# Three of eight score products of a chunk moved ahead of the groups of left-over rows, and the queries split one chunk sooner on VectorE

## The reference

```
a2k     = softmax(scale * agents @ k^T)        # 49 x 12480
agent_v = a2k @ v                              # 49 x 128
q2a     = softmax(scale * q @ agents^T)        # 12480 x 49
x       = q2a @ agent_v                        # 12480 x 128
```

## Time and profile before

| | us |
|---|---|
| median of 3 runs | 885.77 |
| the runs | 885.68 to 885.78 |
| the profiled execution | 886.51 |
| its span in the trace | 884.8 |

### The profile page before, as it was taken

One profiled execution on the slowest core, in us unless ns is written; L12 is line 12 of the kernel. 1 busy time (PEld: TensorE's weight loads), 2 busy tenths in 40 slices (PEclk: granted clock), 3 DMA queues, 4 the chain that ended last, 5 costly groups with the idle time before them and its releaser, 6 DMA issues.

```text
span 884.8 us, 15670 instructions
## 1 busy us (share of the span) xinstructions
PE 878.8 (99%) x5496; PEld 442.5 (50%) x5496; DVE 671.3 (76%) x984; ACT 551.2 (62%) x763; POOL 144.3 (16%) x139
## 2 busy tenths in 40 slices
PE   9999999999999999999999999999999999999998
PEld 8865555545545454444444444444444444444444
DVE  4888788788877777778777777778778777777765
ACT  2457776767666566566666666666666666666554
POOL 6502222322001100011001011011011011010100
PEclk9999999999999999999999999999999999999999
DMA  9942222222222331121112111112111111121110
GB/s 357 398 134 83 63 65 82 84 64 84 82 88 88 116 119 38 38 61 37 38 39 62 37 41 59 37 42 58 39 47 51 40 56 41 40 62 33 31 36 21
DMA packets 59992, 66.20 MB, mean 75 GB/s; under 512 B 36368, under 2 KB 41904, under 8 KB 58800
## 3 DMA queue, kind: packets, MB, share of 16 engines
q1 hardware_dynamic: 59520, 65.51, 23.8%
q10 hardware_dynamic: 432, 0.16, 0.1%
HBM read 41.60 MB, written 12.78 MB: 61 GB/s over the span
## 4 chain that ended last, share of the span: by engine, by line
PE 96%; DMA 2%; DVE 1%; SPq 0%; ACT 0%; issue 0%; DVEq 0%
PE ps L725 60%; PE ps L696 19%; PE ps L713 7%; PE ps L511 1%; PE ps L664 1%; PE ps L586 1%; PE ps L594 1%; DMA kv_s<-kT 1%; PE ps L740 1%; PE ps L624 1%; DVE r_lo L1462 1%; PE ps L925 1%; PE ps L751 1%; PE ps L541 0%; PE ps L644 0%; PE ps L693 0%
## 5 line engine op out<-in xcount | busy, mean ns | idle before, releaser
L1462 DVE SCALAR_TENSOR_TENSOR r_lo<-ps,r_hi 128x1024 f16<-128x1024 f32 (+1 forms) x392 | 468.4, 1216 | 179.5 <-ACT r_hi L1165 179.1
L1165 ACT ACTIVATE r_hi<-ps 128x1024 f16<-128x1024 f32 (+1 forms) x392 | 388.5, 1017 | 159.0 <-PE ps L713 153.1
L725 PE MATMUL ps<-r_hi,w_hi 128*128 128x512 f16 (+1 forms) x784 | 241.0, 383 | 0.1
L725 PE MATMUL ps<-r_lo,w_hi 128*128 128x512 f16 (+1 forms) x784 | 239.5, 380 | 0.0
L725 PE MATMUL ps<-r_hi,w_lo 128*128 128x512 f16 (+1 forms) x784 | 237.8, 380 | 0.0
L696 PE MATMUL ps<-PT,M_a 128*128 128x512 f16 x768 | 198.1, 379 | 0.2 <-DVE r_lo L1462 0.2
L488 POOL TENSOR_TENSOR y<-y_relu,y_lin 128x512 f32<-128x512 f32 x48 | 78.4, 1632 | 531.9 <-ACT y_relu L1280 326.8
L725 PEld LDWEIGHTS ps<-r_lo,w_hi 128*128 128x128 f16 x784 | 76.7, 98 | 81.9
L696 PEld LDWEIGHTS ps<-PT,M_a 128*128 128x128 f16 x768 | 72.2, 98 | 83.7 <-DVE r_lo L1462 15.2
L725 PEld LDWEIGHTS ps<-r_hi,w_lo 128*128 128x128 f16 x784 | 74.3, 98 | 78.9 <-issue 0.8
L725 PEld LDWEIGHTS ps<-r_hi,w_hi 128*128 128x128 f16 x784 | 63.3, 98 | 89.1 <-issue 41.7
(11 more groups left out here) (180 smaller groups left out, 727.4 us busy)
## 6 DMA issues: line engine op xcount, KB each, us to landing
q_s<-qT SPq DMA_DIRECT2D x48, 256.0 KB, 2.8
out<-y SPq DMA_DIRECT2D x48, 256.0 KB, 2.1
kv_s<-kT SPq DMA_DIRECT2D x23, 512.0 KB, 4.7
kv_s<-vP SPq DMA_DIRECT2D x12, 514.5 KB, 9.9
kv_s<-vS SPq DMA_DIRECT2D x6, 1028.5 KB, 5.3
PR<-PT SPq DMA_DIRECT2D x147, 32.0 KB, 1.8
PT<-stack SPq DMA_TRANSPOSE x196, 2.3
w_lin<-w_out SPq DMA_DIRECT2D x1, 1024.0 KB, 9.1
```

The costliest lines, as they stand in the source:

```text
L725: mm = pe.matmul(ps[:, OUT, 0:wide], w[:, 2 * p + u, :], r[:, s, u, 0:wide], start=(p == 0 and u == 0 and k == 0), stop=(p == PAIRS - 1 an ...
L1165: act.activation(r_hi[:, p % RING, :, 0:wide], ps[:, at:at + 2, 0:wide], ACT.Relu).then_inc(hi_ready, 1)
L1462: dve.scalar_tensor_tensor(out=r_lo[:, p % RING, :, 0:wide], in0=ps[:, at:at + 2, 0:wide], scalar=0.0, in1=r_hi[:, p % RING, :, 0:wide], o ...
```

## The change

In plain chunks for which there are queries to score (24 to 45), steps 0, 1 and 2 leave the second layer. Step 0 goes behind tiles 1 and ahead of group 0, which is in the body of the chunk before; step 1 behind tiles 3, ahead of group 1; step 2 behind tiles 5, ahead of group 2. Steps 3 and 4 stand behind the last two products of second layer 2, steps 5, 6 and 7 behind the first three of second layer 3. Since step 0 now needs `q_12` and `q_rest` a body sooner, DVE makes `q_rest` of chunk n+4 behind `split_shift(n + 3)` in body n, and no longer at the start of body n+1. The number of products and of vector operations is the same.

```diff
+        def at_turns(kind):
+            return kind == PLAIN
+        def next_at_turns(half, kind):
+            return kind == PLAIN or kind == MIX_REST and half == 1
@@ PE
+                    turns = at_turns(kind) and there(n + 3)
+                    def turn_step(step):
+                        if turns:
+                            scored = split_score(step, nb3)
+                            if step == 7:
+                                scored.then_inc(q_scored, 1)
                     def second_group():
                         tiles(2, half, b)
                         pe.wait_ge(lo_ready, g + 1)
                         tiles(3, half, b)
+                        turn_step(1)
                         rest_of_quad(1, half, b)
...
                     tiles(5, half, b)
+                    turn_step(2)
                     rest_of_quad(2, half, b)
...
+                        elif turns:
+                            if t >= 4:
+                                turn_step(t - 1)
                         elif there(n + 3):
                             scores(t)
                     def fourth(t):
-                        if not split:
+                        if turns:
+                            if t < 3:
+                                turn_step(t + 5)
+                        elif not split:
                             scores(t + 6)
...
                         tiles(1, 1 - half, nb)
+                        if next_at_turns(half, kind) and there(n + 4):
+                            scores_read(n + 3)
+                            pe.wait_ge(q_split, n + (5 - AHEAD))
+                            split_score(0, BOTH if is_last(n + 4) else 1)
                         pe.wait_ge(q_spread, 48 * n + 96)
                         rest_of_quad(0, 1 - half, nb)
@@ DVE
-                    if there(n + 3):
+                    if there(n + 3) and not at_turns(kind):
                         query_rest(n + 3, 1 - half)
...
                     elif there(n + 3):
                         split_shift(n + 3)
+                    if next_at_turns(half, kind) and there(n + 4):
+                        query_rest(n + 4, half)
```

## The result

The changed kernel takes 888.47 us in the median of 13 runs (887.82 to 889.71), the kernel before 886.00 (885.68 to 887.56): 2.47 us more, a ratio of 1.0027 with a 95% interval of 1.0018 to 1.0035. Forecast were 2.7 us more. The interval reaches from 1.6 to 3.1 us: clear of no change, and too wide to tell 2.3 us from 2.7. The profiled execution took 888.32 us with a span of 886.6.

The account below looks back on a forecast made before the run. PE bounds the kernel (99% busy, 96% of the chain); +0.16 wait - 0.16 + 0.13 in 20 loop chunks is 2.6 us, plus 0.1 in chunks 44 and 45: +2.7 on 885.77, 888.5 us, range 887.6 to 889.6.

Parts of the forecast that it names:

- The wait at tiles 7: PE's load for tiles 7 waits for `r_lo` of pair 5, 3.99 us behind group 2; the 0.16 removed becomes waiting.
- The price ahead of the groups: Behind tiles 1, 3 and 5 the three moved score products add 0.05 + 0.03 + 0.05 = 0.13 us a chunk.
- The gap of 0.095 ahead of a group: At PE's entry of a group 0.095 us streams nothing; it counts from the last columns, so follows the score products.
- rival a: The gap ahead of a group hides the short products, the added 0.13 is 0: 885.8 us; chance 0.14.
- rival c: Scores ahead of a group cost the gap twice, 0.42 a chunk, 9.2 us: 895, or 890 to 892; chance 0.10.
- Rival (b): Wait for `r_lo` of pair 5 gives way, PE keeps 0.16: alone 885.1, chance 0.06; with hidden products 882.2, 0.08.
- Rival (d): DVE's sooner split holds up `r_lo` of pair 6; a tenth of a microsecond a chunk gives 890.5; chance 0.04.
- In chunks 44 and 45: Behind the loop the release is 0.08 sooner, so PE stands only 0.08: +0.05 each, 0.1 us together.
- Two smaller readings: PE reaches step 0 behind tiles 1 some 4 us after DVE is through; chances within 0.2% sum to 0.22.

Follow-up runs that it names:

- experiment 2: The changed kernel with score steps 0, 1 and 2 left out, that part of the scores not computed: 885.78 us, ratio 1.0000 to the kernel before.
- (3): The changed kernel with the first two products of second layer 4 moved between tiles 6 and tiles 7: 885.15 us, ratio 0.9989 to the kernel before.
- (4): The changed kernel with step 2 back behind the fourth product of second layer 2: 887.42 us, ratio 1.0016 to the kernel before.
- (7): The changed kernel with the loop over chunks 24 to 43 written out: 887.32 us, ratio 1.0011 to the kernel before.
- experiment 1: The DVE part of the change alone, `query_rest` one chunk sooner, all eight score products back in second layers 2 and 3: 886.21 us, ratio 1.0002 to the kernel before.
- experiment 6: The kernel before with its loop over chunks 24 to 43 written out: 886.24 us, ratio 0.9998 to the kernel before.

## Why the prediction was right

**The wait at tiles 7** was the step that decided, and it holds in every number: the stretch stayed 3.99, the load's idle time grew by 0.16, leaving the products out of the changed kernel only gets back what they cost ahead of the groups (experiment 2), filling the place with other work brings the 0.16 back (3), putting one back costs nothing there (4), and a release 0.08 sooner takes the 0.08 off (7).

**The price ahead of the groups** was mis-sized a little: 0.05 + 0.03 + 0.05 = 0.13 forecast, 0.045 + 0.023 + 0.045 = 0.113 found. I had taken the 0.05 from the first score product in the second layer. A reading that fits, and that no run takes apart: that distance holds some 0.005 for the next weight load, which starts late behind a score product (last section), while ahead of a group the load comes late anyway. By that term alone 2.7 us become 20 x 0.113 + 2 x 0.04, or 2.3; the windows give 2.35, and the medians 2.47. The estimate from the Trainium skill ("TensorE: Matmul & The Clock Gate", Back-to-back issue gap) was 0.11, nearer than mine, and this trace agrees with it: the wide product at 0.045 is close to its 0.043, the narrow one at 0.023 to its 0.025.

**The gap of 0.095 ahead of a group** comes after the score product in full, as rows 10 said: neither does it hide the product (rival a) nor does it come twice (rival c). Rival (b) needed a shorter chain; where there was one, in experiment 7, the change cost less (1.3 us) and was still no gain. Rival (d) fell with experiment 1, and by the row: `r_lo` of pair 6 starts 605.56 - 603.98 = 1.58 behind group 3 (its products follow tiles 7 at 603.98), as before.

**In chunks 44 and 45** the forecast was 0.05 more each. At the edges of the loop the windows changed by -0.04 (ahead of chunk 24's linear part, 16.28 to 16.24), +0.04 (chunk 44, 16.29 to 16.33) and +0.09 (the one behind it, 15.88 to 15.97), which is 0.09 for the two.

**That 888.47 falls on the forecast of 888.5** is partly luck. With more runs the median of the kernel before moved from 885.77 to 886.00, 0.23 up, and the change came out 0.23 below the 2.7. The 2.47 itself holds 0.1 that the chunks don't explain and that is within the noise.

**Two smaller readings were off** without a consequence. `q_rest` ends at 604.36 + 0.68 = 605.04 and PE comes to step 0 behind tiles 1 at 607.68, 2.6 us later and not some 4. And the chances of a change within 0.2% add up to 0.14 + 0.06 + 0.03 = 0.23, not 0.22.

## What to carry to other kernels

Before work is taken out of a stretch of the busiest engine, measure the stretch against the chain that runs beside it: here 3.98 us of PE (599.04 to 603.02) stood against 3.99 us of group, ACT and DVE, and each of the three products in between was free. Work moved out of such a stretch costs its full price in its new place; it pays only if other work is put into the hole, as two products of the second layer did. A busy share of 99% on both sides does not show such a hole, the idle time ahead of the weight load does.

## What the runs showed of the hardware

A short float32 product between a product of 512 columns and a group on row strips costs about as much as its columns: 0.045 us for 98 and 0.023 for 50, so 0.022 for the 48 more, and at that pace 98 columns are 0.045. The idle 0.095 us at the entry of a group can't be filled by either. Among products of 512 columns, with others of its kind next to it, it costs more: the distances there are 0.276 for a wide and 0.259 for a narrow one, 0.060 and 0.043 more than 0.216. What goes with it is a late weight load. In the kernel before, ahead of the first score product and behind it:

```profile
600.03 0.10 PEld L725 LDWEIGHTS ps<-r_lo,w_hi 128*128 128x128 f16 x1
600.24 0.19 PEld L664 LDWEIGHTS ps<-agents,q 128*128 128x128 f32 x1
600.50 0.10 PEld L725 LDWEIGHTS ps<-r_lo,w_hi 128*128 128x128 f16 x1
```

The first of these loads stands 0.21 ahead of its product at 600.24, the last only 0.01 ahead of its product at 600.51, about where the score product's columns end (600.24 + 0.216 + 0.045 = 600.50). That the late load is the cause of the higher price is argued from these rows, not tested.

ACT starts on a group's end later in the loop than in written-out code. In the kernel before, group 2 ends at 599.04 + 0.39 = 599.43 and `r_hi` starts at 599.57, 0.13 to 0.14 later. In experiment 6, PE's group and ACT's start:

```profile
614.94 0.39 PE L713 MATMUL ps<-PR,M_r 32*128 32x512 f16 x3
```

```profile
615.38 1.94 ACT L1165 ACTIVATE r_hi<-ps 128x1024 f16<-128x1024 f32 x2
```

615.33 to 615.38 is 0.05. The two programs differ there in that the counts waited for are constants instead of register values. A register value alone doesn't cost it: DVE starts 1.05 to 1.06 behind ACT in both kernels (600.62 - 599.57; 616.44 - 615.38), and PE's load is let go 0.05 behind DVE in both (603.03 - 602.98; 618.85 - 618.80). What sets `relu_hi` on ACT apart is that it waits for two counts in a row, the group (`h_ready`) and a free place for `r_hi` (`pair_done`, L1163). In the trace the register instruction for the second starts at 599.485, 0.05 behind the group's end, and `r_hi` 0.08 behind that; the view of its line gives tenths:

```profile
L1163 ACTq ALU_OP  x1: 35/35/35, 599.5 to 599.5; - x1
```

So in the loop this computing stands behind the first wait, on the chain that decides at tiles 7. No run with the two waits in the other order shows it by itself.
